# Attention by pairs of heads: one load and one split for two heads, operands placed by on-chip transfers, values in two column halves

## The reference

```python
# attention, 16 heads (2 x 8), 768 rows, head_dim 64
q_bits = (einsum('bhsd,dk->bhsk', q, proj) > 0)      # 6 bits; k_bits alike
mask   = q_bucket[:, :, :, None] == k_bucket[:, :, None, :]
scores = where(mask, scale * q @ k.T, -1e9); scores -= scores.max(-1)
attn   = exp(scores) / (exp(scores).sum(-1) + 1e-9)
x      = attn @ v                                    # -> (1536, 512)
# SoLU layer: h = x @ w_in; h * softmax(h); layer norm; @ w_out
# then 8 experts, one per token: relu(x @ w1[e]) @ w2[e], scaled by two gates
```

## Time and profile before

| | |
|---|---|
| median of 3 runs | 755.76 us (753.0 to 756.95) |
| profiled execution, its own time | 755.65 us |
| its span, first to last instruction | 753.7 us |
| mean granted TensorE clock | 0.958 |
| busy share of the span: TensorE, VectorE, ScalarE, GpSimd | 88%, 64%, 46%, 36% |
| first scores | 14.68 us |
| turn_ln of the first token tile | 338.74 us |
| routing and scatter | about 497 to 530 us |

### The profile page before, as it was taken

The page is one execution under the profiler, slowest core; times in us unless marked ns, Lnnn a source line. Parts: engine busy times, 40 slices in busy tenths (PEclk is TensorE's granted clock), DMA queues, the critical chain, the costliest instruction groups (busy, mean ns, idle before and its releaser), DMA issues.

```text
span 753.7 us, 11820 instructions
## 1 busy us (share of the span) xinstructions
PE 665.0 (88%) x3190; PEld 518.8 (69%) x3191; DVE 484.5 (64%) x931; ACT 344.6 (46%) x563; POOL 271.9 (36%) x185
## 2 busy tenths in 40 slices
PE   3899999999999998899999999830599999999994
PEld 1677666666666666668888888620488787787883
DVE  5688888888888889745656656465134647454621
ACT  2566666666666666432222222341325545454510
POOL 2566666666666664432322313537000000001011
PEclk9999999999999999999999999965699999999997
DMA  9933333333333331011000000045534565556400
GB/s 261 283 101 98 99 97 97 97 97 97 97 97 97 97 97 35 1 60 53 1 1 0 0 0 0 26 142 210 184 137 134 205 209 201 199 175 238 146 17 27
DMA packets 35419, 79.48 MB, mean 105 GB/s; under 512 B 6461, under 2 KB 6589, under 8 KB 35392
## 3 DMA queue, kind: packets, MB, share of 16 engines
q1 hardware_dynamic: 28112, 67.97, 28.5%
q10 hardware_dynamic: 5040, 4.87, 2.4%
q0 software_dynamic: 2240, 6.31, 2.2%
HBM read 67.82 MB, written 12.35 MB: 106 GB/s over the span
## 4 chain that ended last, share of the span: by engine, by line
PE 67%; DVE 15%; issue 8%; POOL 3%; ACT 3%; DMA 2%; DVEq 1%; ACTq 1%; SPq 0%; POOLq 0%
PE PS L456 8%; PE PS L439 7%; PE PS L418 7%; DVE sb_nm L681 4%; PE PS L612 4%; PE PS L614 4%; PE PS L613 4%; PE PS L524 3%; PE PS L593 3%; PE PS L471 3%; PE PS L473 3%; PE PS L472 3%; PE PS L595 3%; PE PS L594 3%; PE PS L526 3%
## 5 line engine op out<-in xcount | busy, mean ns | idle before, releaser
L1200 POOL TENSOR_TENSOR at_P<-at_P,sb_rr 128x768 f32<-128x768 f32 x80 | 120.2, 1511 | 111.0 <-DVE sb_rr L693 109.0
L456 PE MATMUL PS<-at_PT,at_V 128*128 128x384 f32 x384 | 133.9, 486 | 0.0
L991 ACT ACTIVATE at_P<-PS,sb_nb,sb_sc 128x768 f32<-128x768 f32 x96 | 95.7, 997 | 61.6 <-DVE sb_nb L685 61.6
L916 DVE TENSOR_TENSOR at_W<-at_raw,at_W 128x2048 f32 (+1 forms) x29 | 65.7, 2290 | 70.6 <-ACT at_W L1070 68.0
L681 DVE TENSOR_REDUCE sb_nm<-PS 128x1 f32<-128x768 f32 x96 | 91.6, 954 | 23.6 <-PE PS L418 23.5
L418 PE MATMUL PS<-at_B,at_A 128*128 128x384 f32 x384 | 98.0, 380 | 9.0 <-POOL at_B L1211 5.8
L456 PEld LDWEIGHTS PS<-at_PT,at_V 128*128 128x128 f32 x384 | 72.2, 190 | 38.4
L1005 ACT ACTIVATE at_PT<-PS 128x384 f32<-128x384 f32 x160 | 66.7, 491 | 60.2 <-PE PS L439 59.9
L439 PE MATMUL PS<-sb_cst,at_P 128*128 128x128 f32 x576 | 79.2, 282 | 15.0 <-DVE at_P L697 6.6
L1293 POOL DMA_INDIRECT out<-at_yb,sb_to x16 | 15.8, 985 | 205.3 <-DVE at_yb L928 205.3
L439 PEld LDWEIGHTS PS<-sb_cst,at_P 128*128 128x128 f32 x576 | 65.8, 143 | 33.0 <-issue 13.7
(11 more groups left out here) (148 smaller groups left out, 1176.0 us busy)
## 6 DMA issues: line engine op xcount, KB each, us to landing
at_raw<-w SPq DMA_DIRECT2D x32, 1024.0 KB, 5.3
at_AA<-qT SPq DMA_DIRECT2D x32, 192.0 KB, 4.0
at_KK<-kT SPq DMA_DIRECT2D x32, 192.0 KB, 4.3
at_V<-vP SPq DMA_DIRECT2D x16, 384.0 KB, 3.1
rows_by_expert<-at_empty SPq DMA_DIRECT2D x19, 257.0 KB, 10.8
at_XS<-rows_by_expert ACTq DMA_DIRECT2D x17, 256.0 KB, 2.7
at_stg<-w_solu SPq DMA_DIRECT2D x16, 256.0 KB, 3.4
at_QK<-qT SPq DMA_DIRECT2D x16, 192.0 KB, 3.8
```

What stands on the lines that cost most here:

```text
L456: m = mm(PS[:, PVB, 0:UQ], V[c][:, kt, :], PTb[w][:, kt, :], start=(kt == 0), stop=(kt == KT - 1))
L991: fn(Pr[w][j % UT].rearrange("p (g n) -> p g n", g=2), slot(7 * c + 1 + j), ACT.Exp, bias=nb[:, col], scale=sc[:, col], accum_out=sm[:, co ...
L1200: pool.tensor_tensor(p, p, rr[:, col].broadcast_to([P, S]), ALU.mult).then_inc(s_norm, 1)
```

## The change

- Heads are loaded, hashed and split in pairs. `load` brings q and k of two heads (64 + 64 partitions) in Rq and Rk, once. `high_parts` rounds both in two instructions to Hq and Hk; `low_parts` on GpSimd subtracts in place, after the hashes have read Rq and Rk.
- `fill` places the operands of each head by ten transfers from SBUF to SBUF: six of 64 x 768, and four of 12 x 384 for the bits.
- `hashes` makes four products, each in a column group of 32 of the array, in bank HSB, which is also the third bank of the transposes. One VectorE instruction, `hash_bits`, makes all bits of the pair.
- `values` makes each product in two column halves: 64 columns of V, half of the window's rows in each, to partitions 0 to 63 and 64 to 127 of one bank. `attended` copies once a head, in two instructions, and comes a head later.
- Scores go up to eight tiles ahead of the transposes. There are two sets of tiles Pr, one for each head of a pair.
- `inverse` takes three tiles at once; GpSimd normalises all six.
- The weights of the SoLU layer are scaled first, on VectorE (`weights_scaled`), then rounded on ScalarE (`weights_high`), then subtracted on GpSimd (`weights_low`). 
- In the routing, `low_chunk(2)` goes from GpSimd to VectorE.

```diff
-            pe.wait_ge(s_setup, 1)
-            hashes(0, 0, True)
-            for j in range(UT + 1):
-                scores(0, 0, j, True)
+            pe.wait_ge(s_setup, 1)
+            hashes(0)
+            for j in range(TILES):
+                scores(0, 0, 0, j)
+            for j in range(2):
+                scores(1, 1, 0, j)
+            hashes(1)
+            pe.wait_ge(s_bits, 2)
...
+            def load(p):
+                wait(sp, ld_f[0], FILL * p)
+                wait(sp, ld_f[1], FILL * p)
+                for r, x in ((Rq, qT), (Rk, kT)):
+                    sp.dma_start(r, x[ds(p, 1)].rearrange("o d s -> d (o s)")).then_inc(ld_r, 16)
+
+            def fill(h, c, p):
+                wait(sp, s_low, p + 1)
+                wait(sp, s_bits, p + 1)
+                wait(sp, s_slot, 6 * h - 6)
+                mine = slice(c * D, (c + 1) * D)
+                for to_, src in ((A1[c][0:D], words(Hq[mine])), (A1[c][D:P], words(Hq[mine])), (A2[c][0:D], Rq[mine]),
+                                 (B1[c][0:D], words(Hk[mine])), (B1[c][D:P], Rk[mine]), (B2[c][0:D], words(Hk[mine]))):
+                    sp.dma_start(words(to_), src).then_inc(ld_f[c], 16)
+                for g in range(2):
+                    at_g = slice(g * HALF, (g + 1) * HALF)
+                    r = 2 * g * GROUP + c * BITS
+                    for to_, r_ in ((A2[c], r), (B2[c], r + GROUP)):
+                        sp.dma_start(words(to_[D:D + BITS, at_g]), words(HB[r_:r_ + BITS, :])).then_inc(ld_f[c], 16)
...
+            def hashes(p):
+                wait(pe, ld_r, 32 * p + 32)
+                wait(pe, s_bits, p)
+                for g in range(2):
+                    for n, r in ((0, Rq), (1, Rk)):
+                        t = (2 * g + n) * GROUP
+                        m = mm(PS[t:t + GROUP, HSB, 0:HALF], hashw[:, n * GROUP:(n + 1) * GROUP],
+                               r[:, g * HALF:(g + 1) * HALF], start=True, stop=True)
+                m.then_inc(s_hash, 1)
...
+            def values(h, c, p, w):
...
+                for kt in range(KT):
+                    for g in range(2):
+                        m = mm(PS[g * D:(g + 1) * D, PVB, w * QQ:(w + 1) * QQ], V[c][:, kt, :],
+                               PTb[w][:, kt, g * QQ:(g + 1) * QQ],
+                               start=(kt == 0), stop=(kt == KT - 1))
+                m.then_inc(s_pv, 1)
```

The new order in TensorE's queue, for head h with c = h % 2:

```diff
+                    if more:
+                        scores(h + 1, 1 - c, p1, 2)
+                    transposes(h, c, 0, (0, 1, 2))
+                    if more:
+                        scores(h + 1, 1 - c, p1, 3)
+                    else:
+                        hidden(0, 0, 0, True)
+                    if c == 1:
+                        values(h - 1, 0, i, 1)
+                    elif not (isinstance(i, int) and i == 0):
+                        values(h - 1, 1, i - 1, 1)
+                    if more:
+                        scores(h + 1, 1 - c, p1, 4)
+                    transposes(h, c, 0, (3, 4, 5))
+                    if more:
+                        scores(h + 1, 1 - c, p1, 5)
+                    transposes(h, c, 1, (0, 1, 2))
+                    if left > 0:
+                        scores(h + 2, c, i + 1, 0)
+                    elif c == 1:
+                        hidden(0, 0, 1, True)
+                    values(h, c, i, 0)
+                    if c == 1 and left > 1:
+                        pe.wait_ge(*evac_count(2, h, 1))
+                        hashes(i + 2)
+                    if left > 0:
+                        scores(h + 2, c, i + 1, 1)
+                    transposes(h, c, 1, (3, 4))
+                    if c == 1 and left > 1:
+                        pe.wait_ge(s_bits, i + 3)
+                    transposes(h, c, 1, (5,))
```

VectorE's and ScalarE's orders, and what the new instructions are (GpSimd: normalize of window 0 of the next head, weights_low, normalize of window 1, and after each pair low_parts):

```diff
 VectorE
+                    if more:
+                        maximum(h + 1, 1 - c, 2)
+                        maximum(h + 1, 1 - c, 3)
+                        inverse(h + 1, 1 - c, 0)
...
+                        attended(i, h - 1, 0)
...
+                    if more:
+                        maximum(h + 1, 1 - c, 4)
+                    turned(h, 0, 5)
+                    weights_scaled(h, c)
+                    if more:
+                        maximum(h + 1, 1 - c, 5)
+                    turned(h, 1, 2)
+                    if left > 0:
+                        maximum(h + 2, c, 0)
+                    if more:
+                        inverse(h + 1, 1 - c, 1)
+                    if c == 1 and left > 1:
+                        hash_bits(i + 2)
+                    if left > 0:
+                        maximum(h + 2, c, 1)
+                    turned(h, 1, 5)
...
+            def weights_scaled(m, c):
+                wait(dve, ld_w[c], 8 * m + 16 - 8 * c)
+                dve.tensor_scalar(stg[c], stg[c], gcol[:, ds(m, 1)], None, ALU.mult).then_inc(s_ws, 1)
 ScalarE
+                    for kt in (0, 1, 2):
+                        turned(h, 0, kt)
+                    if more:
+                        weights_of(h + 1, 1 - c, 2)
+                        weights_of(h + 1, 1 - c, 3)
...
+                    weights_high(h, c)
+                    for kt in (3, 4):
+                        turned(h, 0, kt)
+                    if more:
+                        weights_of(h + 1, 1 - c, 4)
+                    for kt in (0, 1):
+                        turned(h, 1, kt)
+                    if more:
+                        weights_of(h + 1, 1 - c, 5)
+                    if left > 0:
+                        weights_of(h + 2, c, 0)
+                    for kt in (3, 4):
+                        turned(h, 1, kt)
+                    if left > 0:
+                        weights_of(h + 2, c, 1)
+                    if c == 1 and left > 1:
+                        high_parts(i + 2)
...
             def weights_high(m, c):
-                wait(act, ld_w[c], 8 * m + 16 - 8 * c)
-                fn(piece(m, 0), stg[c], ACT.Copy,
-                   scale=gcol[:, ds(m, 1)]).then_inc(s_wh, 1)
+                wait(act, s_ws, m + 1)
+                fn(piece(m, 0), stg[c], ACT.Copy).then_inc(s_wh, 1)
```

More of the change, by code:

```diff
@@ L747, in soft @@
                                   ALU.mult).then_inc(m_dv, 1)
-            hash_rows(0, 0)
-            key_high(0, 0)
-            for j in range(UT + 1):
+            dve.wait_ge(s_w, 16)
+            hash_bits(0)
+            for j in range(4):
                 maximum(0, 0, j)
-                if j:
-                    inverse(0, 0, j - 1)
-            def heads(i, first, last):
+            inverse(0, 0, 0)
+            for j in (4, 5):
+                maximum(0, 0, j)
+            maximum(1, 1, 0)
@@ L757, in heads @@
+            inverse(0, 0, 1)
+            maximum(1, 1, 1)
+            hash_bits(1)
+            def heads(i, left):
                 for c in range(2):
                     h = 2 * i + c
-                    f = first and c == 0
-                    end = last and c == 1
-                    turned(h, 0, 0, f)
-                    inverse(h, c, 3)
-                    maximum(h, c, 4)
-                    maximum(h, c, 5)
-                    inverse(h, c, 4)
-                    if not end:
-                        key_high(h + 1, 1 - c)
@@ L1060, in heads @@
[L1060 to L1065 removed]
+                    more = left > 0 or c == 0
+                    for kt in (0, 1, 2):
[4 more added lines that the diff above has]
+                    else:
+                        act.wait_ge(s_pvev, HEADS // 2)
+                        take(0, 0, 0, True)
```

436 lines of the change are left out of this document (176 added, 260 removed).

## The result

The changed kernel takes 788.5 us (median of four, 785.5 to 791.1) where the kernel before took 756.1 on the same chip: ratio 1.0455, 95% interval 1.042 to 1.049. I had said 768, 735 to 800, and 0.58 for slower. The sign and the mechanism came as forecast; the size did not: 32 us where I had 12.5. The profiled execution took 788.34, its span 786.5. One execution of the second kernel of experiment 10 took 3588.75 us and is left out of its figures.

What follows compares the result with a forecast made beforehand. TensorE was taken to carry attention, VectorE close behind. Terms to the first turn_ln summed to 354.1 us against 338.7, 15.4 later; less 2.9 for routing, 12.5 more: 768 us, range 735 to 800.

Steps and rivals of the forecast that it cites:

- start, to the first body: Loads, hashes, operands and eight score tiles before the first body: first scores at about 22, 41.3 us in all.
- 14 bodies with hashes and operands: Attention loop: 14 bodies of 17.4 us, six hash turns 9.6, and seven times 1.65 for the operands.
- body 15 to turn_ln: Last attention body up to turn_ln, with an idle gap of nearly 5 us and low clock behind it: 32 us.
- behind it, against before: Routing after turn_ln: low_chunk(2) moved to VectorE gains 4.1 less 1.2, so 2.9 us.
- the one that matters: In each body, ScalarE's weights_high waits for VectorE's weights_scaled, which ends at 8.35 or 9.5 to 9.6; wait 3 to 4 us.
- my walk: One attention body followed through all four engines from scores(h+1, 2): closes at 15.7 or 16.9, taken as 16.3 us.
- Once a pair: the operands: high_parts, low_parts and ten transfers for the next pair of heads: 0.15 survives plus 1.5 stall, 1.65 us a pair.
- The stall at the transfers: scores(h+2, 0) waits for the last of ten operand transfers: 1.3 to 2.8 us or none, taken as 1.5.
- The clock: TensorE's idle gap in each body lowers its clock: 1.1 us a body, bounds 0 and 1.7.
- C: Rival: the two column halves of values do not overlap; body 19.0, total 811 us; chance 0.15.
- B: Rival: clock holds and weights_scaled gets in ahead of the third normalise; body 15.7, total 740 us; chance 0.28.
- TensorE carries the stage: Premise on attention in the kernel before: TensorE, busy 95.3 of 100 us, sets its pace, VectorE close behind.

Runs made afterwards that it cites:

- experiment 10: Values' records issued one column half after the other: in the changed kernel 803.9 us; second kernel, the same edit on that of experiment 6, 738.6 us.
- Experiments 1: Changed kernel with weights_high moved later in ScalarE's queue, behind exp 4 and window 1's first two evacuations: 756.8 us, ratio 1.004 to the kernel before.
- experiment 7: Changed kernel with weights_scaled moved up in VectorE's order, in front of maximum 4: 759.5 us, ratio 1.010 to the kernel before.
- Experiment 9: Changed kernel with high_parts moved from the end of the odd body to just before weights_high: 795.7 us, ratio 1.056 to the kernel before.
- experiment 4: Kernel before with only its values in two column halves, and attended in two copies for them: 756.4 us, ratio 1.003.
- experiment 6: Changed kernel with weights_high later in ScalarE's queue and the ten operand transfers issued in the order their sources are ready: 714.3 us, ratio 0.950.

## Why the prediction had the direction and not the size

The sum of the prediction against the trace, in us up to the first turn_ln:

| step | forecast | measured | difference |
|---|---|---|---|
| start, to the first body | 41.3 | 38.55 | -2.8 |
| 14 bodies with hashes and operands | 264.8 | 285.4 | +20.6 |
| body 14 | 16 | 16.2 | +0.2 |
| body 15 to turn_ln | 32 | 35.6 | +3.6 |
| to turn_ln | 354.1 | 375.8 | +21.7 |
| behind it, against before | -2.9 | -4.3 | -1.4 |

**The mechanism was right.** The step that I called the one that matters was: ScalarE stands in front of weights_high for weights_scaled, 3.9 us in an odd body (3 to 4 forecast), and TensorE's second half began at 10.42, where my walk gave 9.7 or 10.9. Experiments 1 and 7 take the wait away on either side and win 31 and 27 us. My walk left open whether weights_scaled would get in ahead of the third normalise. It did not: in the odd body shown the normalises ended at 151.29 and weights_scaled at 151.57, in the even one at 171.83 and 172.11, 0.28 behind in both.

**The odd bodies were sized right**: 18.6 against 17.4 and 1.6 for the hashes, 19.0. The hashes took 0.85 and not 1.6: I took the stagger of two halves for them, but four column tiles run side by side: eight records in 0.85, where four took 1.29 before. The body without them was 0.4 longer than 17.4.

**The step that failed is "Once a pair: the operands", 1.65 us a pair, which was 4.45** (12.33 - 10.42, 3.12 - 1.36 and 5.14 - 4.36). It makes 2.8 x 7 = 19.6 of the 20.6 us; the rest is about 0.4 in each of 14 bodies less 0.8 in each hash turn. It failed in three places:

- "0.15 of that survives, the rest lies under weights_scaled": 1.9 survived. I had let high_parts push exp 2 and stopped there. But behind exp 2 stands VectorE's inverse, and behind the inverse stand GpSimd's normalises, with which weights_scaled ends, and VectorE's own attended, maximum 4 and evacuation, so the push moves the very thing that was to cover it. The inverse starts 5.42 us into the even body and 4.19 into the odd one: 1.2. And its first instruction, three columns wide, took 0.84 instead of 0.16 (L723 in the two timelines), ending at 167.23 with GpSimd's low_parts (167.20): 0.7 more. I had both, the end of low_parts at 6.25 into the body (it was 6.23) and the lock, and did not put them together. Experiment 9 gives the push its price: without it the gap ends up to 1.9 us sooner.
- The stall at the transfers: 1.5 forecast, 1.76 here. The parts moved: SyncE needed 7.7 us for ten issues and not 5.5, since the four small ones took 0.71 to 0.95 each and not 0.43 to 0.5; the last one, issued from 174.33, was there at most 2.1 us later, where I had bounds of 2.5 and 4.
- The clock: I had charged it once a body. In the even body the second wait lies inside the low stretch and makes it longer (scores and values 0.8 us more than in the odd one, clock 0.57 from 174 to 182).

**The end, 3.6 more.** hidden(0) runs mostly at half clock behind its wait, records 0.43 apart, not 0.23, and so does hidden(1): twelve records in 5.1 us. I had charged the clock there once. **The start, 2.8 less**: the first scores stood at 21.12 and not 22, and of the eight tiles two ran at full clock, where I had taken half speed throughout and 1.5 more in body 0.

**The rivals.** C (no overlap) is refuted by the 2.17 window and by experiment 10: 24 records one half after the other make 0.147 each, alternating ones 0.090. The Trainium skill, "TensorEngine Tiling (Array Packing)", Key Properties, has tiles independent, and draining between modes; the trace agrees with the first, and shows no cost of the second: the values start at 145.10, where the scores before them end at 145.18. B (weights_scaled gets in ahead of the normalise) did not occur in the changed kernel, but experiment 7 shows something near it: weights_scaled in 0.47 us ahead of the second normalise, and an odd body of 14.7.

**One premise fell**: "TensorE carries the stage". It did no harm to the sum, which was made by a walk through the handovers, but it hid that the kernel before gains nothing from faster values (experiment 4).

What stays open: which wait takes up the other 1.9 of the 5.4 us in experiment 10, and what holds the even body of experiment 6 at 15.5, 1.2 above the odd one. The push of high_parts is still in it, and no run took it out there; the trace shows scores(h+1, 4) 5.45 us into the even body and not 4.73, and a wait of 1.02 before the last transposes ahead of scores(h+2, 0), for VectorE's evacuation. Open too is the one even body of 26.7 us in experiment 6.

## What to carry to other kernels

When work moves to another engine, look at which instruction then waits for it and at everything queued behind that instruction; here a conversion of weights that only the next stage reads held the evacuations of every head, and moving it down its queue won 31 us. A push is not absorbed by a wait unless the thing waited for stays where it is: follow the push through the releaser too. And an engine at 95% is the bound only if shortening its work shortens the time; a run that does just that costs one edit.

Of several transfers on one queue, those whose sources are ready first should be issued first: that order alone was worth 20 us of 736.

## What the runs showed of the hardware

- Where a VectorE instruction between SBUF buffers (L729, L723) began while one of GpSimd's ran, it did not end before it, whatever its size: 8 columns took 0.88 and 1.32 us and 3 columns 0.84, each ending 0.03 behind GpSimd's; 512 columns took 1.13 and 1.57, ending 0.28 behind, and 0.48 at 90.95 in the changed kernel, where GpSimd was idle. In experiment 7, at 102.33, VectorE's fell on the seam of two of GpSimd's and took 0.47, and GpSimd's second took 1.88 instead of 1.47. A small instruction of statistics was hit as hard as a large one.
- Transfers inside the chip cost SyncE no less to issue when small: from 167.33 to 175.04, 12 rows of 384 took 0.71 to 0.95 us each, 64 rows of 768 0.59 to 0.93, and the ten in a row held the queue for 7.7 us.
- TensorE's clock: behind a gap of 2.9 us the granted clock was 0.61 from 154 to 158; behind a gap of 4.2 us, with a second pause of 1.6 in the low stretch, it was 0.57 from 174 to 182. At 1.00 a window of values took 2.17 us, in these two stretches 2.85 and 3.64.
- Column tiles of fp32: two halves of 24 records in 2.17 us, one after another 3.52; four quarters, 8 records of 384 columns, in 0.85.
